# Attention and two expert mixtures on one core: opening stage reordered, last output tile laid over all partitions, token table moved to GpSimd

## The reference

```
attention: B=4, 8 heads, 576 positions, head size 64; heads 0-3 see the last 32 keys,
           heads 4-7 every 4th of the last 128; softmax, times v      -> x (4, 576, 512)
mixture 1: logits = x @ w_gate (4 experts), the best 2 with softmax weights;
           each expert is a causal attention (x@wq, x@wk, x@wv, @wo), summed by weight -> x
mixture 2: logits = x @ w_gate (8 experts), local_gate = sigmoid(x @ w_local)
           e = argmax(logits) if s == 0 or local_gate < 0.5 else e of the token before
           out[token] = softmax(logits)[e] * (relu(x @ w1[e]) @ w2[e])
```

## Time and profile before

| | us |
|---|---|
| median of 3 runs | 718.95 |
| lowest, highest | 718.87, 719.3 |
| profiled execution, its own time | 713.36 |
| span of the profiled execution | 711.6 |
| PE busy | 700.3 |
| DVE, ACT, POOL busy | 303.6, 288.3, 97.4 |

### The profile page before, as it was taken

The page is one execution under the profiler, slowest core; times in us unless marked ns, Lnnn a source line. Parts: engine busy times, 40 slices in busy tenths (PEclk is TensorE's granted clock), DMA queues, the critical chain, the costliest instruction groups (busy, mean ns, idle before and its releaser), DMA issues.

```text
span 711.6 us, 15586 instructions
## 1 busy us (share of the span) xinstructions
PE 700.3 (98%) x5239; PEld 518.4 (73%) x5240; DVE 303.6 (43%) x916; ACT 288.3 (41%) x865; POOL 97.4 (14%) x138
## 2 busy tenths in 40 slices
PE   8999999999999999999999999999999999999997
PEld 8888777687676877776666777777676767777774
DVE  3854887158861788416657311112111211122111
ACT  3853778257872677614620223222322232222320
POOL 3310001000100001000022121112111221112113
PEclk9999999999999999999999999999999999999999
DMA  8783127330372213300026135611440770001101
GB/s 180 168 209 80 35 60 199 102 67 2 94 201 66 68 23 101 111 7 1 31 79 240 31 106 206 221 67 40 143 157 29 265 283 29 29 30 39 43 29 38
DMA packets 86467, 69.59 MB, mean 98 GB/s; under 512 B 69102, under 2 KB 69118, under 8 KB 86416
## 3 DMA queue, kind: packets, MB, share of 16 engines
q1 hardware_dynamic: 78816, 44.73, 22.5%
q0 software_dynamic: 7600, 24.19, 10.0%
HBM read 118.12 MB, written 11.27 MB: 182 GB/s over the span
## 4 chain that ended last, share of the span: by engine, by line
PE 96%; DVE 2%; ACT 1%; issue 1%; POOL 0%; ACTq 0%; DVEq 0%; POOLq 0%
PE bank L1314 22%; PE bank L1325 21%; PE bank L812 9%; PE bank L808 5%; PE bank L903 5%; PE bank L733 5%; PE bank L862 4%; PE bank L891 4%; PE bank L773 4%; PE bank L711 3%; PE bank L833 3%; PE bank L746 2%; PE bank L704 2%; PE bank L1297 1%; PE bank L700 1%; PE bank L838 1%
## 5 line engine op out<-in xcount | busy, mean ns | idle before, releaser
L1314 PEld LDWEIGHTS bank<-pt,stage_b 128*128 128x128 f32 x1344 | 155.0, 192 | 10.0 <-issue 10.0
L1325 PE MATMUL bank<-w_all,raw_all 128*128 x352 | 158.2, 593 | 0.0
L1314 PE MATMUL bank<-pt,stage_b 128*128 128x128 f32 x1344 | 156.9, 275 | 0.0
L1789 ACT ACTIVATE raw_all<-bank 128x512 f32<-128x512 f32 x44 | 26.3, 597 | 214.3 <-PE bank L1314 214.3
L1325 PEld LDWEIGHTS bank<-w_all,raw_all 128*128 128x128 f32 x352 | 63.6, 191 | 63.6 <-issue 63.6
L2388 DVE TENSOR_SCALAR raw_all<-bank,p_slot 128x512 f32 x21 | 15.8, 751 | 208.9 <-PE bank L1325 208.9
L625 POOL DMA_INDIRECT out_dram<-raw_all,idx_out x25 | 37.7, 1506 | 246.7 <-DVE raw_all L2388 229.8
L812 PE MATMUL bank<-stage_b,w_all 128*128 128x288 f32 x256 | 69.0, 415 | 0.6 <-issue 0.6
L1505 ACT ACTIVATE pr<-sm,negmax_a 96x80 f32<-96x80 f32 (+1 forms) x168 | 59.8, 359 | 3.2 <-DVE negmax_a L1841 3.1
L812 PEld LDWEIGHTS bank<-stage_b,w_all 128*128 128x128 f32 x256 | 46.3, 190 | 16.3 <-issue 5.2
L1494 ACT COPY w_sb<-bank 128x256 f32<-128x256 f32 (+5 forms) x93 | 37.6, 421 | 27.3 <-PE bank L862 25.9
(11 more groups left out here) (231 smaller groups left out, 902.4 us busy)
## 6 DMA issues: line engine op xcount, KB each, us to landing
w_sb<-in_moe_w_dram SPq DMA_DIRECT2D x19, 2048.0 KB
w_all<-in_moe_w_dram SPq DMA_DIRECT2D x19, 2048.0 KB
w_sb<-in_moe_w_dram POOLq DMA_DIRECT2D x12, 512.0 KB, 4.8
w_all<-in_moe_w_dram POOLq DMA_DIRECT2D x12, 512.0 KB, 4.7
mixture_rows<-y_sb SPq DMA_DIRECT2D x16, 256.0 KB, 2.1
raw_all<-in_q_dram SPq DMA_DIRECT2D x28, 144.0 KB
raw_all<-in_k_dram SPq DMA_DIRECT2D x28, 144.0 KB
v_dil<-in_v_dram SPq DMA_DIRECT2D x42, 80.0 KB, 3.4
```

The source lines that it names most:

```text
L1314: last = pe.matmul(ps[half][:, f * P:(f + 1) * P], w1_sb[:, 0, c * F + at:c * F + at + P] if buf is None else w1_fix[:, c, at:at + P], xT[ ...
L1325: last = pe.matmul(ps[5], hidT[:, half * HALF + n * P:half * HALF + (n + 1) * P], w2_sb[:, bass.ds(buf, 1), half, n * D:(n + 1) * D].rearr ...
```

## The change

1. **Opening.** 11 `turn_over` instead of 24 ahead of the first `pe_use`; the band matmul moves behind the second `pe_use` (and its copy on ACT with it); behind that place up to the first projection there are 17 `turn_over` in place of 19, most of them further back. The hand-written orders of `pe_first`, `act_first` and `dve_first` are changed: scores of group 1 go behind two more pieces, `pe_router_turn` goes from behind group 8's probabilities to behind group 2's, and the eight `pe_router` matmuls are spread one by one.
2. **Loads.** wo and the two router weights are issued ahead of v of pairs 2 and 3.
3. **Last output tile.** The 64 tokens of tile 4 are computed as two halves of 256 columns, the second on partitions 64 to 127: four matmuls of 256 columns for two of 512, one copy of 128x256 for one of 64x512, two stores for one.
4. **Routing.** The sum, the addition and the reciprocal of the softmax go behind the scan; the base of each expert is read from the scan's own output, shifted by one column, so that a subtraction falls away; `token_hot` is made by POOL instead of DVE; the row index is written as integers by the operation that computes it, so that a cast falls away. Two `turn_over` groups lose 3 and 2 of their matmuls, the two between the parts of the product go from 3 and 3 to 2 and 0. The late part of the tables has one more operation of 25 columns.

```diff
@@ SP's loads
-            load_v(sp, 0, 2)
-            load_v(sp, 0, 3)
             sp.dma_start(wo_sb, wo.rearrange("(x e) d n -> (e d) x n", e=2)).then_inc(router_loaded, 16)
...
+            load_v(sp, 0, 2)
+            load_v(sp, 0, 3)
@@ POOL, behind its waits for the stores
             pool.sem_inc(rows_stored, 1)
+            pool.wait_ge(reach_ready, 1)
+            pool.tensor_tensor(token_hot, reach, c_token[:, :].unsqueeze(2).broadcast_to([P, LT, SLOTS + 1]), ALU.mult
+                               ).then_inc(token_hot_ready, 1)
             pool.wait_ge(row_ready, 1)
@@ pe_out
+            n = D * nq // P
             for p in range(PAIR_E):
-                last = pe.matmul(X[0:nq, :], OT[:, p, T0[t]:T0[t] + nq], wo_sb[:, p, :],
-                                 start=(p == 0), stop=(p == PAIR_E - 1))
+                for r in range(0, P, nq):
+                    c0 = r // nq * n
+                    last = pe.matmul(X[r:r + nq, 0:n], OT[:, p, T0[t]:T0[t] + nq], wo_sb[:, p, c0:c0 + n],
+                                     start=(p == 0), stop=(p == PAIR_E - 1))
@@ PE, routing
             pe_out(pe, B - 1, None, NT - 1, TR)
-            turn_over(pe, ps[6], 3)
             product(3)
...
-            turn_over(pe, ps[6], 5)
+            turn_over(pe, ps[6], 3)
             product(4)
...
                 if t % HOT == 0:
-                    turn_over(pe, ps[0], 3 if t > 0 else 0)
+                    turn_over(pe, ps[0], 2 if t == HOT else 0)
@@ dve_route
-            dve.wait_ge(route_exp, 1)
-            red(r1[2][:, :], ex, ALU.add)
-            ts(r1[2][:, :], r1[2][:, :], EPS, ALU.add)
-            step(v_.reciprocal(r1[5][:, :], r1[2][:, :]))
             dve.wait_ge(keep_moved, 1)
             dve.wait_ge(route_product, 2)
             tell(v_.tensor_tensor_scan(seq[:, 0:S], keep, bank[1][0:B, 0:S], 0.0, ALU.mult, ALU.add))
+            dve.wait_ge(route_exp, 1)
+            red(r1[2][:, :], ex, ALU.add)
+            ts(r1[2][:, :], r1[2][:, :], EPS, ALU.add)
+            step(v_.reciprocal(r1[5][:, :], r1[2][:, :]))
...
-            tt(e8[2][:, :], e8[1][:, :], e8[0][:, :], ALU.subtract)
-            stt(in_expert, along(e8[2][:, :], LT), float(P), count[:, :, 0:LT], ALU.mult, ALU.add)
+            stt(in_expert, along(e9[1][:, 0:EF], LT), float(P), count[:, :, 0:LT], ALU.mult, ALU.add)
...
-            v_.tensor_tensor(token_hot, reach, along(c_token[:, :], SLOTS + 1), ALU.mult).then_inc(token_hot_ready, 1)
...
-            ts(idx_f[:, 0, 0:SLOTS], tok[:, 0:SLOTS], -1.0, ALU.add, 0.0, ALU.max)
-            v_.tensor_copy(idx[:, 0, :], idx_f[:, 0, :]).then_inc(row_ready, 1)
+            v_.tensor_scalar(idx[:, 0, 0:SLOTS], tok[:, 0:SLOTS], -1.0, 0.0, ALU.add, ALU.max).then_inc(row_ready, 1)
```

More of the change, by code:

```diff
@@ L191, in build @@
         e8 = [sb(f"e8_{i}", [P, EF]) for i in range(4)]
+        e9 = [sb(f"e9_{i}", [P, EF + 1]) for i in range(2)]
+        per_expert, slots_to = e9[0][:, 1:], e9[1][:, 1:]
         tab = sb("tab", [1, 5, SLOTS + 1])
@@ L970, in pe_first @@
             pe_scores(pe, a, 6)
             pe_values(pe, a, 1)
-            turn_over(pe, O2, 4)
+            pe_use(pe, None, a, 11, 0)
+            pe_probs(pe, a, 2)
+            pe_router_turn(pe, None)
+            pe_values(pe, a, 2)
             pe_probs(pe, a, 3)
+            pe_scores(pe, a, 7)
             pe_use(pe, None, a, 12, 0)
+            pe_values(pe, a, 3)
+            pe_probs(pe, a, 4)
             pe_use(pe, None, a, 13, 0)
-            pe_values(pe, a, 2)
-            pe_probs(pe, a, 4)
```

178 lines of the change are left out of this document (94 added, 84 removed).

## The result

| | before | after |
|---|---|---|
| median of the timed runs, us | 719.12 (718.87 to 719.37, 4 runs) | 705.99 (705.02 to 707.1, 4 runs) |
| ratio | | 0.9818 [0.9801, 0.9835] |
| profiled execution, its own time | 713.36 | 706.34 |
| its span | 711.6 | 704.6 |

Two numbers do not fit together. The medians differ by 13.1 us, the two profiled executions by 7.0, less than my sum of 10.2. To read any number of this case one must know that both kernels run at one of several times, by how long TensorE is granted its lower level in that run: the profiled execution of before had a mean granted clock of 0.999, but two thirds of its 86 runs beside the experiments were under 0.993.

The account below looks back on a forecast made before the run. PE's queue was taken to set the pace. Opening -4.5, last output tile -2.8 and routing -2.9 summed to -10.2 us, taking the median from 718.95 to 708.8 us, range 707.3 to 711.9.

Parts of the forecast that it names:

- my sum of 10.2: Whole kernel: savings of 4.5 us in the opening, 2.8 in the last output tile and 2.9 in routing.
- I keep the distance: Whole kernel: the timed median stays 5.6 us above the profiled execution, so 718.95 - 10.2 = 708.8 us.
- Opening to the first scores: PE's start: fewer `turn_over` save 4.05 us, band matmul gives back 0.71; first scores 3.35 us earlier.
- From the scores to the projection: Rest of the opening: three fewer `turn_over` and no 0.56 us wait save 1.33 us, less 0.2 for short waits.
- the rival of the late load: Opening: router weights need 23 to 25 us, or first q lands late; some 2 us lost, 710.8; chance 0.15.
- Last tile: Tile 4's `pe_out`: two halves run at the same time, 1.0 us for 1.93, saving 2.8 over three batches.
- Routing: Routing stage: scan 0.35 us earlier, `reach` 1.5, product 1.55, row index 2.9, which all behind it follows.
- the lock: Routing, DVE against POOL: `low_hot`'s first part waits out POOL's table multiplication until 374.8; without it 0.25 us better.
- The rival of the late table: Routing: POOL not free by 374.1 waits out all of `low_hot`; product 2.4 us later, 711.2; chance 0.15.
- the clock rival: Opening: TensorE stays at its lower level up to the router matmuls, costing 12.4 us, kernel at 721.0; chance 0.03.

Follow-up runs that it names:

- e8: The changed kernel, unedited, run again: median 707.44 us, ratio 0.985 to the kernel before.
- e13: The changed kernel, unedited, run a third time on another chip: median 705.1 us, ratio 0.9815 to the kernel before.
- e5: The kernel before with only the eight opening `pe_router` matmuls spread one by one and the copies of their results moved behind: median 713.0 us, ratio 0.9934.
- e11: The changed kernel with the old front again (24 `turn_over` and the band matmul at PE's start): median 707.57 us, ratio 0.9839 to the kernel before.
- e9: The changed kernel with wo and the router weights loaded ahead of q and k of pair 3: median 705.1 us, ratio 0.9806 to the kernel before.
- e14: The kernel before with the new front alone (11 `turn_over`, band matmul behind the second piece), router row kept: median 715.59 us, ratio 0.9952.
- e7: The changed kernel with the token table made by DVE again instead of POOL: median 704.87 us, ratio 0.9825 to the kernel before.
- e3: The kernel before with the routing part of the change alone: median 716.81 us, ratio 0.999.
- e2: The kernel before with the last output tile's part of the change alone: median 714.47 us, ratio 0.9953.
- e6: The changed kernel with the eight `pe_router` matmuls put back in a row: median 706.05 us, ratio 0.9852 to the kernel before.
- e16: The changed kernel with early router loads and the eight `pe_router` matmuls back in a row: median 710.98 us, ratio 0.9881 to the kernel before.
- e12: The kernel before with one `turn_over` added between each two of the eight `pe_router` matmuls, seven in all: median 716.92 us, ratio 0.9977.
- e15: The changed kernel with early router loads, token table on DVE and last-batch logits spread, second run: median 704.45 us, ratio 0.9811 to the kernel before.

## Why the prediction was wrong, step by step

**The step that failed: "I keep the distance".** I took the 5.6 us between the profiled execution and the median for a constant that goes along. It was, for the most part, the price of a clock that fell in most timed runs and not in the profiled one. The changed kernel's median lies 0.35 us below its profiled execution (705.99, 706.34), so 5.76 + 0.35 = 6.1 us of the 13.1 come from there. The experiments' own share for the clock is a little smaller: beside e8 and e13 the median of before lies 4.6 and 5.3 us above its high runs, and the high runs of the two kernels lie 8.6 and 8.3 apart. e5 removes the falls with one edit to the kernel before. My sum was of PE's records at a clock of 1.00, and the earlier trace rows could not have shown the falls. The hint was the distance itself: a median 5.6 us above one execution, with three runs within 0.4 us, is not noise. I had the clock as a rival only as a loss at the start of the program. No rival of mine had it as a gain.

**Opening to the first scores: 2.74 for 3.35.** The mechanism was right, the term too large. The first piece starts at 6.73, not 6.53, and the first 32 records take 1.69 us where the next 32 take 1.22, with PE busy in both: 0.47 us of the slow records, which were all `turn_over` before, now falls on real work. (The windows print a clock of 1.00 there, as they do over the 421 ns records of the earlier trace rows, so this is read from the durations.) The band matmul costs 0.78 from its start to the next record, where I had 0.71. That is 0.74 us of loss; 0.13 came back elsewhere. One pair of profiles doesn't measure this well: with the old front the first scores stand at 13.2 to 14.5 us in the profiles, with the new one at 10.0 to 11.4, by how early the records turn fast. The timed runs have the front at 2.5 us (e11 against e9) and 2.75 to 3.1 (e14), below my 3.35 too.

**From the scores to the projection: 0.0 for 1.13** (1.33 less the 0.2 for short waits). This is the rival of the late load: I had it issued at 16.8 and landed at 21.7 by 4.9 us. It was issued at 17.98 and took 5.8. PE wanted it at 23.1, a microsecond later than I had it, and stood until 23.86. I had given that rival a chance of 0.15 although my margin was 0.3 us, a term read from one row. e9 and e11 show 1.0 of it to be there once the load is in time.

**Last tile: 2.45 for 2.8.** The halves run at the same time as in the earlier trace rows: eight records in 1.08 us for four in 1.93. At 1.0 my figure was a little low; the sum over three batches is 2.55 by the records and 2.45 by the shift of the stage (49.89 to 47.16 against 364.89 to 359.71 at the transposes of the routing).

**Routing: 2.4 for 2.9 at the row index, 1.8 at the end.** Against its stage's start the scan came 0.30 earlier (forecast 0.35), `reach` 1.2 (1.5), the product 1.0 (1.55), the row index 2.4 (2.9). Half of the miss is `reach`. The rest is the lock, which I had on the wrong instruction: POOL's multiplication began at 368.73 and took 1.06 (I had 1.2), but what waited it out was the small operation on the rank. A cast still had to follow it, and so `low_hot` started at 370.06, 0.27 behind POOL's end, at full speed (2.96 for all three, as before), where I had it waiting and running on at once. The profiled execution then gave back 0.56 us between the product of the probabilities and ACT's copy of it, a wait that e9's profile has again and e8's and e13's have not; so it belongs to an execution and not to the change. The Trainium skill, "SBUF — State Buffer", section "Who interferes with whom", counts `tensor_scalar`, where its operands meet certain conditions, among the operations that can contend with GpSimd for the shared port pair, and says that whoever issues first holds it for the whole instruction. The traces agree on the contention: in seven profiles the small operation stands beside POOL's multiplication and ends 0.02 to 0.05 us behind it; it took 0.18 in e7 and e9, where it doesn't stand beside it. On the order one of them doesn't fit: in e3 the operation's record began 0.45 us ahead of POOL's and yet lasted to POOL's end, 1.57 us. I had read that section for the two-input multiplication only.

**The rival of the late table had its price wrong.** I had POOL wait out all three parts of `low_hot`, +2.4 us. In e9 POOL was late, released by the last store of y:

```profile
367.51 3.83 DVE L2280 TENSOR_TENSOR stage_b<-c_row,r 128x1024 f32<-128x1024 f32 x3
367.56 2.10 POOL L613 TENSOR_TENSOR stage_b<-stage_b,c_token 128x520 f32<-128x520 f32 x1 [0.98 <-DMA mixture_rows<-y_sb]
```

The first part of `low_hot` took its usual 1.22 us and POOL's multiplication 2.10; then the second part took 2.09. Each waited for one instruction of the other and not for all of them. The product started 9.58 us behind the scan, in the changed kernel 9.61: it cost nothing. (A slip beside it: the sum for the clock rival, 708.8 + 12.4, is 721.2 and not 721.0.)

**The sum.** 2.73 + 2.45 + 1.82 = 7.0 us between the profiled executions, where I had 10.2: each term too large, by 1.8, 0.35 and 1.1. The median was further down all the same. Had the clock not changed, my 708.8 would have been too low, by 3 us if the profiled pair is the measure and by 1.6 to 1.9 if the high runs are (8.3 to 8.6 us apart). Which of the two is nearer stays open. Two errors of opposite sign came out as one of 2.8; that it is no larger is luck.

## What to carry to other kernels

Before a sum is made against a profile, ask whether the median and the profiled execution are the same kind of run: the mean granted clock of each timed run says it at a glance, and a distance of 0.8% is a term to be explained. Sixteen records of 9 columns in a row kept PE busy in the profile, and yet the clock fell at them in every profile of a low run that has the row (e2, e3, e6, e14, e16); spread such narrow matmuls among others. Where a shorter prologue overtakes a load, the load's row must be read with a wide margin (here it landed 2.1 us later than worked out), and the load moved with it.

## What the hardware showed that I had not expected

- The clock fell to its lower level with PE busy throughout: at sixteen records of 9 columns in 1.9 us (profiles of e2, e3, e6, e14, e16), and at twelve in 1.5 us (e3, e6, e8, e14, e16). It stayed there 3.4 us in e8 and 13.7 in e2. With two records at a time between other matmuls no run of twelve had a clock under 0.998 (e5).
- It is a matter of chance with one and the same program: 58 of 86 runs of before fell under 0.993, 23 kept 0.998 or more.
- At the start TensorE rises at different moments: the first 24 records of `turn_over` took 5.36 us in the profile of before and 4.55 in those of e11 and e12; the same early part of e9, e15 and e16 put the first scores at 10.79, 10.00 and 10.39.
- A DVE operation of 20 columns on integers took 1.04 us instead of 0.18 while POOL multiplied (0.94 to 1.57 in the seven profiles that have it so).
- A POOL multiplication of two inputs of 520 columns took 1.06 us. By the figure in the Trainium skill, "GPSIMD Engine Reference", section 3.1, it was an estimated 1.14; the trace agrees.
